# Softmax sums taken off the probabilities and put on the attention output, with kept weight slices and a one-instruction leaky step

## The reference

```
scores = q @ k.T / 8          # per head
keep   = (key < 4) or (0 <= row - key < 128)
a      = exp(scores - max);  a = a / (sum(a) + 1e-9)
x      = a @ v                # reshaped to 1536 tokens x 512
h = x @ w_in;   g = max(0.01 * h, h);   x = g @ w_out      # first layer, 512 -> 2048 -> 512
h = x @ w_in2;  g = h * sigmoid(h);     y = g @ w_out2     # second layer
```

## Time and profile before

| | us |
|---|---|
| median of 3 runs | 679.57 (679.01 to 680.44) |
| profiled execution, span from the first to the last instruction | 677.8 |
| PE busy | 634.3 |
| DVE busy | 415.4 |
| ACT busy | 362.4 |
| GpSimd busy | 99.3 |

### The profile page before, as it was taken

How to read it: one execution, slowest core, us unless ns; L and a number is a source line. 1 busy time by engine, 2 the same in 40 slices (tenths; PEclk the granted TensorE clock), 3 DMA queues, 4 the chain that set the end, 5 groups by cost and what they waited for, 6 DMA issues and landing times.

```text
span 677.8 us, 9233 instructions
## 1 busy us (share of the span) xinstructions
PE 634.3 (94%) x3048; PEld 529.2 (78%) x3048; DVE 415.4 (61%) x894; ACT 362.4 (53%) x788; POOL 99.3 (15%) x133
## 2 busy tenths in 40 slices
PE   2566799999999999999999999999999999999997
PEld 2565678888887778888888888888888888888886
DVE  7999977888888887886654545333343333433332
ACT  4667766666667666664544446443344434443342
POOL 5544422222324232200000000000000000000000
PEclk9977799999999999999999999999999999999999
DMA  6343981211121120000222221000010000100001
GB/s 145 110 113 111 297 261 34 47 48 33 48 47 33 48 63 17 1 1 1 93 94 93 94 94 31 1 0 1 1 62 1 0 1 1 58 6 0 1 1 62
DMA packets 12334, 36.50 MB, mean 54 GB/s; under 512 B 2048, under 2 KB 2048, under 8 KB 12288
## 3 DMA queue, kind: packets, MB, share of 16 engines
q1 hardware_dynamic: 12288, 35.92, 18.1%
HBM read 32.77 MB, written 3.15 MB: 53 GB/s over the span
## 4 chain that ended last, share of the span: by engine, by line
PE 62%; DVE 22%; ACT 8%; issue 6%; DMA 1%; ACTq 0%; SPq 0%; DVEq 0%
PE y_ps L808 29%; PE h_ps L781 29%; DVE sm L515 4%; DVE prob L597 4%; DVE pT L524 3%; DVE g_f L559 3%; ACT g L428 2%; ACT g_f L417 2%; DVE g L569 2%; DVE x L537 2%; DVE psT L529 1%; DVE row_inv L590 1%; PE o_ps L748 1%; ACT prob L355 1%; ACT win L400 1%
## 5 line engine op out<-in xcount | busy, mean ns | idle before, releaser
L781 PE MATMUL h_ps<-x,win 128*128 128x512 f32 x1152 | 284.0, 391 | 0.5 <-DVE win L544 0.5
L781 PEld LDWEIGHTS h_ps<-x,win 128*128 128x128 f32 x1152 | 212.8, 188 | 42.6 <-DVE win L544 0.8
L808 PE MATMUL y_ps<-g,wout 128*128 128x512 f32 x576 | 145.7, 393 | 0.0
L808 PE MATMUL y_ps<-wout,g 128*128 128x512 f32 x576 | 138.2, 389 | 0.0
L569 DVE TENSOR_TENSOR g<-g_f,g 128x512 fp32r<-128x512 f32 x96 | 70.9, 739 | 91.7 <-ACT g L421 85.4
L551 DVE TENSOR_TENSOR wout<-w_raw,wout 128x512 fp32r<-128x512 f32 x96 | 72.4, 754 | 86.9 <-ACT wout L408 86.7
L808 PEld LDWEIGHTS y_ps<-wout,g 128*128 128x128 f32 x576 | 108.1, 188 | 22.5
L808 PEld LDWEIGHTS y_ps<-g,wout 128*128 128x128 f32 x576 | 103.9, 188 | 18.6
L408 ACT ACTIVATE wout<-w_raw 128x512 fp32r<-128x512 f32 x96 | 60.2, 627 | 90.9 <-PE y_ps L808 90.9
L355 ACT ACTIVATE prob<-sm,neg_max 128x260 f32<-128x260 f32 x96 | 48.7, 508 | 43.3 <-DVE neg_max L515 42.7
L419 ACT ACTIVATE g_f<-h_ps 128x512 f32<-128x512 f32 x48 | 28.7, 598 | 69.3 <-PE h_ps L781 69.3
(11 more groups left out here) (72 smaller groups left out, 507.2 us busy)
## 6 DMA issues: line engine op xcount, KB each, us to landing
w_raw<-w SPq DMA_DIRECT2D x32, 512.0 KB, 3.5
qk_raw<-qk SPq DMA_DIRECT2D x48, 260.0 KB, 4.2
v_raw<-vt SPq DMA_DIRECT2D x12, 256.0 KB, 2.6
y<-qk_raw SPq DMA_DIRECT2D x12, 256.0 KB, 2.2
vs_raw<-vsink SPq DMA_DIRECT2D x8, 8.0 KB, 3.5
```

The costliest lines, as they stand in the source:

```text
L781: ins = mm(h_ps[:, :], win[:, F % 2, wp, c * P:(c + 1) * P], x[:, xp, c, i * BLK:(i + 1) * BLK], start=(c == 0 and wp == HI and xp == HI), ...
L808: ins = mm(y_ps[d][:, :], a[:, d * P:(d + 1) * P], r, start=(f == 0 and wp == HI and gp == HI), stop=(f == FT - 1 and wp == LO))
```

## The change

- The probabilities are no longer scaled. `exp` writes its sums of four heads side by side; for each half tile DVE adds 1e-9 and takes the reciprocal of the four columns, written 64 times each (128x256). PE turns that into two 128x128 blocks, in the same bank as the turned sinks; DVE copies them to SBUF (`scale`), and multiplies the output bank by them into `att` (`scale_half`). ACT rounds `att` into `x`, and GpSimd takes the low part. The high part of the turned sinks moves from ACT to DVE.
- The first tile of each batch element (tiles 0 and 6) has only its own 128 key columns: its scores, masks, exps, transposes and products leave out the rest. Tiles 0 and 1 of each element have no separate sink products.
- Weight slices are split into a store of eight slots. A block goes through the slices in the opposite order of the one before, so that the last eight of a block are still there: 64 splits instead of 96. The raw slices come through a ring of four buffers, one load per split.
- Leaky: ACT applies Prelu with slope 0.01 twice from the bank, as it does Silu in the second layer; `leaky` and `round_g` are gone.
- The first layer step is placed at tick 19 instead of 20, and the orders on all engines are written anew.

```diff
+        if F % FT < FT - KEPT or b == NB - 1:
+            del resident[layer, f]
+            free.append((split_slot[j], F))
...
+        if s < FT:
+            at, at_out = s - 4, s - 3
+        elif i < FT - KEPT:
+            at = at_out = s - 6
+        else:
+            i -= FT - KEPT
+            at = start + 2 + i + i // 2
+            at_out = at + 1
...
-            def normalise(u):
-                dve.wait_ge(exp_done, 2 * u + 2)
-                at = (2 * u) % PR
-                nc.vector.tensor_scalar_add(row_inv[:, u % 2, 0, :], row_sum[:, at:at + 2],
-                                            1e-9).then_inc(norm_step, 1)
-                dve.wait_ge(norm_step, 2 * u + 1)
-                nc.vector.reciprocal(row_inv[:, u % 2, 1, :], row_inv[:, u % 2, 0, :]).then_inc(norm_step, 1)
-                dve.wait_ge(norm_step, 2 * u + 2)
-                for i in range(2):
-                    a = prob[:, at + i, :]
-                    nc.vector.tensor_scalar(a, a, row_inv[:, u % 2, 1, i:i + 1], None,
-                                            ALU.mult).then_inc(prob_ready, 1)
...
+            def take_half(e):
+                k = job["half", e]
+                dve.wait_ge(t_written, k + 1)
                 bank_ = t_bank(k)
+                if has_sinks(e // 2):
+                    wait(dve, o_done, e)
+                    nc.vector.tensor_copy(psT[:, :], bank_[:, 2 * P:3 * P]).then_inc(sink_step, 1)
+                nc.vector.tensor_copy(scale[:, :, :], bank_[:, 0:2 * P].rearrange("p (c n) -> p c n", c=2)).then_inc(
+                    scale_ready, 1)
+                if has_sinks(e // 2):
+                    dve.wait_ge(sink_step, sunk(e) + 1)
+                    low = psT[P // 2:P, :]
+                    ins = nc.vector.tensor_tensor(low, bank_[P // 2:P, 2 * P:3 * P], low.bitcast(F32), ALU.subtract)
+                    ins.then_inc(t_ready, 1)
                 else:
+                    dve.wait_ge(scale_ready, e + 1)
+                    dve.sem_inc(t_ready, 1)
+            def invert_sums(e):
+                dve.wait_ge(exp_done, 4 * (e + 1))
+                wait(dve, t_written, job["half", e - 1] + 1 if e else 0)
+                nc.vector.tensor_scalar_add(sum_eps[:, :], row_sum[:, e % 2, :], 1e-9).then_inc(norm_step, 1)
+                dve.wait_ge(norm_step, 2 * e + 1)
+                nc.vector.reciprocal(row_inv[:, :, :],
+                                     sum_eps[:, :].unsqueeze(2).to_broadcast([P, H // 2, D])).then_inc(norm_step, 1)
+            def scale_half(e):
+                dve.wait_ge(o_done, e + 1)
+                dve.wait_ge(scale_ready, e + 1)
+                wait(dve, x_ready, e)
                 for lo in (0, D):
+                    src = o_bank(e)[lo:lo + D, :].rearrange("p (c n) -> p c n", c=2)[:, :, 2 * lo:2 * lo + P]
+                    ins = nc.vector.tensor_tensor(att[lo:lo + D, :, :], src, scale[lo:lo + D, :, :], ALU.mult)
+                ins.then_inc(att_ready, 1)
...
             def take_hidden(F):
+                func, slope = (ACT.Prelu, 0.01) if F < N_L0 else (ACT.Silu, 0.0)
                 act.wait_ge(h_done, F + 1)
                 wait(act, g_ready, F - 1)
+                nc.scalar.activation(g_f32[:, F % 2, :], h_ps[:, :], func, alpha=slope)
                 wait(act, y_done, F - 1)
+                nc.scalar.activation(g[:, 0, F % 2, :], h_ps[:, :], func, alpha=slope).then_inc(h_taken, 1)
...
+            def turn_half(e):
+                k = job["half", e]
+                wait(pe, t_ready, freed(t_bank, k))
+                pe.wait_ge(norm_step, 2 * e + 2)
+                bank_ = t_bank(k)
+                for c in range(2):
+                    src = row_inv[:, 2 * c:2 * c + 2, :].rearrange("p h d -> p (h d)")
+                    ins = nc.tensor.transpose(bank_[:, c * P:(c + 1) * P], src, ident[:, :])
+                if has_sinks(e // 2):
+                    pe.wait_ge(sinkp_ready, sink_at[2 * e + 1] + 1)
+                    src = prob_sink[:, e % 2, :, :, :].rearrange("p r h s -> p (r h s)")
+                    ins = nc.tensor.transpose(bank_[:, 2 * P:3 * P], src, ident[:, :])
+                ins.then_inc(t_written, 1)
...
+            for a in range(LAST):
+                head = a < FS
+                F = a - FS
+                if head:
+                    mask_max(2 * a)
+                    mask_max(2 * a + 1)
+                if a in inverted_in:
+                    invert_sums(inverted_in[a])
+                if 2 <= a <= NPAIR + 1:
+                    low_pair(a - 2)
+                if not head and a < NPAIR:
+                    mask_max(2 * a)
+                if a in turned_in:
+                    take_half(turned_in[a])
+                if a in scaled_in:
+                    scale_half(scaled_in[a])
+                if a == 4:
+                    stack_sink_values()
+                if a == FS:
+                    low_g(0)
+                if not head:
                     evacuate(F - 1, 1)
+                    if a < NPAIR:
+                        mask_max(2 * a + 1)
+                for s in wout_in.get(F, ()):
+                    low_wout(s)
+                if not head:
                     low_g(F + 1)
+                for s in win_in.get(F, ()):
+                    low_win(s)
+                if not head:
                     evacuate(F, 0)
...
+                if a < NPAIR:
+                    scores(2 * a)
+                if a == FS:
+                    hidden(0, 0)
+                    hidden(0, 1)
+                hidden(F + 1, 0)
+                if a in turned_in:
+                    turn_half(turned_in[a])
+                hidden(F + 1, 1)
+                if a < NPAIR:
+                    scores(2 * a + 1)
+                if a <= NPAIR + 1:
+                    weigh_values(a - 2)
+                project(F, 0)
+                if a <= NPAIR:
+                    turn_pair(a - 1)
+                if a in turned_in and has_sinks(turned_in[a] // 2):
+                    weigh_sinks(turned_in[a])
+                project(F, 1)
```

More of the change, by code:

```diff
@@ L54, in sink_window_attention_two_ffn @@
     SCALE = 1.0 / float(D) ** 0.5
-    LEAD = TB + 1
     REP = P // (H * NS)
-    assert D == 64 and HD == 512 and REP == 4 and window <= P and NS <= P and NF >= 2
-    job = {}
[L61 to L68, removed]
+    BLK = 512
+    TB = BLK // P
@@ new lines, in has_sinks @@
+    def has_sinks(T):
+        return T % TPB >= 2
+    NHALF = NPAIR // 2
+    sink_pairs = [u for u in range(NPAIR) if has_sinks(u // PAIRS)]
+    sink_at = {u: i for i, u in enumerate(sink_pairs)}
+    turned_in = {2 * e + 3: e for e in range(NHALF)}
+    inverted_in = {2 * e + 2: e for e in range(NHALF)}
+    scaled_in = {2 * e + 4: e for e in range(NHALF)}
+    job = {}
+    for a in range(LAST):
+        if a in turned_in:
+            job["half", turned_in[a]] = len(job)
+        if 1 <= a <= NPAIR:
+            job["pair", a - 1] = len(job)
@@ L130, in freed, with tokens @@
             return next((k + 1 for k in range(i - 1, -1, -1) if bank_of(k) is bank_of(i)), 0)
-        w_loaded = [sem(f"w_loaded{f}") for f in range(FT)]
+        def tokens(F):
+            b = steps[F][1]
+            return slice(b * BLK, (b + 1) * BLK)
+        w_loaded = [sem(f"w_loaded{r}") for r in range(RING)]
         qk_loaded = [sem(f"qk_loaded{i}") for i in range(2)]
@@ L225, in _ @@
                             sp.dma_start(vs_raw[r * n:(r + 1) * n, b, :], vsink[b]).then_inc(vs_loaded, 16)
[L226 to L253, removed]
+                if PAIRS <= a < 2 * PAIRS:
+                    load_w(a - PAIRS)
+                load_ws(a - FS)
+            for F in range(LAST - FS, NSTEP):
+                load_ws(F)
+                i, f = divmod(F - N_L0, FT)
+                if i > 0 and f == 1:
+                    store(i - 1)
+            store(NB - 1)
             for t in range(TB):
@@ L332, in _ @@
             low_v(0, 0)
-            for u in range(NPAIR + 1):
+            for u in range(LAST):
                 T, j = divmod(u, PAIRS)
@@ L375, in high_v, with high_pair @@
                 nc.scalar.activation(v_hl[:, T % TPB % 2, 0, part], v_raw[:, part], ACT.Copy).then_inc(v_high, 1)
-            def high(kind, i):
-                k = job[kind, i]
+            def high_pair(u):
+                k = job["pair", u]
                 act.wait_ge(t_written, k + 1)
[L380 to L386, removed]
@@ L744, in weigh_values @@
                 if u % 2 == 0:
-                    wait(pe, x_ready, freed(o_bank, e))
-                for s in range(2):
+                    wait(pe, att_ready, freed(o_bank, e))
+                only = not has_sinks(T)
+                slots = (0,) if width(T) == P else (0, 1)
+                for s in slots:
                     for vp, pp in PASSES:
```

584 lines of the change are left out of this document (261 added, 323 removed).

## The result

The changed kernel takes 689.84 us (median of 4 runs, 688.40 to 690.53) against 679.44 for the kernel before, measured beside it (4 runs, 679.01 to 680.44): a ratio of 1.0148, 95% interval 1.0136 to 1.0160. It is slower by 10.4 us, where the forecast was 665 and the range ended at 680. The span of the profiled execution is 688.3 against 677.8. A few executions of this and later comparisons ran far slower, at 811 us and more; medians leave them out.

A forecast was written before the change was run, and what follows sets the result against it. DVE was taken to bound the head, PE the rest: first layer product at 75.5, layers 522.2, attention 57.1, losses 5.0, stores 3.8, outside 1.8, together 665 us; range 654 to 680.

The forecast's parts named there:

- the losses behind it: PE's waits after the first layer product: 2 us at the handover and 0.2 per two ticks, 5.0 (3.5 to 11).
- the place of the reciprocal in DVE's even tick: DVE's reciprocal, low pT, mask, scaling: done at some 2.8 us, before PE wants the output bank at 3.4.
- the tick of the head as a sum of DVE's instructions: Head, before layer products: DVE's work gives 6.4 us per two ticks; first layer product at 75.5, 10.5 earlier.
- r: Time of DVE's 128x256 reciprocal of the sums: 1.4 us taken, ends 0.42 and 2.2.
- that rival: Output bank's return, decided by DVE's even-tick chain from r = 2.2 or equal loss beside GpSimd; 0.4 more: 688; chance 0.12.
- Beginning in tick 19 brings no gain of its own.: First layer step one tick earlier: a tick only goes from the head's 3.9 us to PE's 1.9.
- Kept slices "by itself worth nothing": Layer steps after 15 split half the weight slices; no gain, since ACT and DVE are not the bound there.
- the doubled weight transfers are hidden: Weights fetched 64 times instead of 32, hidden by three ticks or more of lead; uncovered, some 3 us a slice.
- Prelu needs no further table: ACT's leaky step; rival: two table loads of 1.28 us per tick, 671 to 740; chance 0.05 with the rest.
- PE's own budget: PE's attention work from the first layer product on: 57.1 us, beside 522.2 of layer products.
- The narrow tiles: Tile 6 at its own 128 key columns saves PE 2.6 us; tile 0's four head ticks take 2.6 each.
- nothing there is due within two ticks: SP's queue: sink loads move behind tile 1's first half, weight loads to ticks 4 to 7, without a near deadline.

The follow-up runs named there:

- the short one on DVE and ACT: Changed kernel with DVE's reciprocal of 128x4 and ACT copying it out to 128x256, first layer step at tick 19: 671.11 us; with tick 20, 668.21.
- The best version: Changed kernel with a 128x4 reciprocal on DVE, its copy to 128x256 on ACT, and the first layer step at tick 20: 668.21 us, ratio 0.9833.

## Why the prediction was wrong

By the forecast's own sum, the first product came at 81.6 instead of 75.5, which is 6.1 us, and the losses behind it were 684.44 - 81.61 - 522.2 - 57.1 = 23.5 us where 5.0 stood, which is 18.5. Together they are the 24.6 by which PE ended too late. The two steps that failed are the place of the reciprocal in DVE's even tick, and the tick of the head as a sum of DVE's instructions. The late reciprocal in the mixed ticks alone brings the losses from 23.5 to 12.9; with the short one on DVE and ACT and the start at tick 20 they are 5.4 (660.31 - 77.48 - 522.2, less 55.2 for one tick fewer).

**The place of the reciprocal: the step that failed.** I wrote "PE wants it 3.4 us into the even tick, DVE is done at some 2.8 for r up to 1.4", and put the point from which DVE's chain decides at r = 2.2. The reciprocal's duration was between my ends, and for this shape the rows read (count, ns min/median/max, start to end):

```profile
L563 DVE RECIPROCAL row_inv<-sum_eps x24: 1752/1753/1755, 13.2 to 318.2; 128x256 f32<-128x256 f32 x24
```

r = 1.75, not 1.4. The even tick of the changed kernel, at 129.64 on PE (timeline, all engines):

```profile
129.19 0.85 POOL L335 TENSOR_TENSOR v_hl<-v_raw,v_hl 128x256 fp32r<-128x256 f32 x1 [5.07 <-ACT v_hl L423]
129.36 0.71 DVE L561 TENSOR_SCALAR sum_eps<-row_sum 128x4 f32<-128x4 f32 x1
129.64 0.33 PE L695 MATMUL s_ps<-k_hl,q_st 128*128 128x128 f32 x2
130.10 1.75 DVE L563 RECIPROCAL row_inv<-sum_eps 128x256 f32<-128x256 f32 x1
131.78 0.63 DVE L535 TENSOR_TENSOR pT<-t_ps,pT 128x512 fp32r<-128x512 f32 x1
132.32 0.28 DVE L527 CUSTOM_DVE_ANT_0 sm<-s_ps,mask 128x128 f32<-128x128 f32 x1
132.52 0.85 DVE L572 TENSOR_TENSOR att<-o_ps,scale 64x256 f32<-64x256 f32 x2
132.64 0.40 ACT L404 ACTIVATE prob<-sm,neg_max 128x128 f32<-128x128 f32 x1 [3.53 <-DVE neg_max L527]
132.75 0.41 PE L695 MATMUL s_ps<-k_hl,q_st 128*128 128x128 f32 x2
133.52 0.71 PE L740 MATMUL o_ps<-pT,v_hl 128*128 128x256 f32 x4 [0.36 <-DVE att L572]
```

The scaling ends at 133.37, 3.7 us after the tick's first scores. That is my 2.8, if two terms are put right: 0.35 for r, and 0.55 because the addition takes 0.71 beside GpSimd instead of 0.16. PE wanted the bank at 133.16, 3.5 after the scores, close to my 3.4. So the place and both quantities were in the text, the addition's wait too ("with as much lost beside GpSimd"), but I set the threshold for the reciprocal alone and gave the case 0.12. The threshold was also miscounted: 2.8 at r = 1.4 reaches 3.4 at r = 2.0 and not 2.2, and at 2.2 the scaling would be 0.2 late and not 0.4. I also priced it by the bank alone. The listed wait for it is only 2.2 us; the same chain delays the low pT that the turning bank waits for (3.1 us), and the mask, for which ACT's exp waits 3.53 us here. With the chain freed, those waits go together, and 10.7 us with them. The 688 of that rival is near what happened, but its parts are not: r at 2.2 with 0.4 more puts the first product at 86.7 and the losses at 17, and they were 81.6 and 23.5. That the sum came close is luck.

The Trainium skill (VectorE: DVE Perf Modes, the pipeline's walkthrough) gives reciprocal a repeat count of 8, from which I estimated 2.1 us above the fixed part; the trace has 1.6 (1753 less 166 ns). The page's figure led to 0.5 us too much, my middle reading to 0.35 too little.

**The head.** Two ticks were 5.0 + r = 6.75 with the true r (my terms add up to 5.1); from mask to mask the rows have 46.09 to 53.11, 7.02. That sum was nearly right. Tick 8 begins at 35.80 and not 34.3, which is the first two tiles, and tick 15 at 60.13 and not 56.7: of the further 1.9, 1.2 are r. From there I had 18.8 us to the first product, four ticks with a slice of 4.5 and 0.8, and it took 21.5. DVE's first masks of these ticks and of tick 19 come at 60.13, 64.58, 71.29, 75.62 and 85.39: the odd ticks have about my 4.5, the even ones, with the reciprocal, have not (6.7 and 9.8). PE's clock was low here (0.51 from 70 to 75 us), but PE did not set the pace: it waited for DVE. Tick 16, of 6.7 us:

```profile
65.77 1.75 DVE L563 RECIPROCAL row_inv<-sum_eps 128x256 f32<-128x256 f32 x1
67.99 0.84 DVE L572 TENSOR_TENSOR att<-o_ps,scale 64x256 f32<-64x256 f32 x2
68.12 1.65 PE L740 MATMUL y_ps<-pT,v_hl 128*128 128x256 f32 x6 [3.80 <-DVE pT L535]
68.86 0.42 ACT L435 ACTIVATE x<-att 128x256 fp32r<-128x256 f32 x1 [2.71 <-DVE att L572]
69.19 0.61 ACT L447 ACTIVATE wout<-w_raw 128x512 fp32r<-128x512 f32 x1
69.83 0.81 DVE L584 TENSOR_TENSOR wout<-w_raw,wout 128x512 fp32r<-128x512 f32 x1 [1.00 <-ACT wout L447]
70.57 0.69 DVE L578 TENSOR_TENSOR win<-w_raw,win 128x512 fp32r<-128x512 f32 x1
71.29 0.43 DVE L527 CUSTOM_DVE_ANT_0 sm<-y_ps,mask 128x260 f32<-128x260 f32 x1
```

The work goes round a ring in which each engine takes its instructions in order: DVE scales, ACT rounds `x` and only then the slices, DVE subtracts the slices and only then begins the next mask. ACT idles 2.71 us in it, DVE 1.00, PE 3.80. I had added up DVE's instructions; in such a tick that is only a lower bound.

**"Beginning in tick 19 brings no gain of its own."** It brings a loss: 3.7 us with the long reciprocal, 2.9 with the short one. The block's first step then waits for a chain over DVE, ACT and GpSimd in its own tick (3.6 us in two blocks, and 1.5 more at the low clock behind the first), and the handover takes 15.1 us for what costs PE 10.1 (a step and a half, 8.2, and a tick's 1.9). Of the 5.0 between them 3.0 are a wait and some 1.6 the 3.2 us at half the clock behind it. There the wait is for ACT, which is held by an exp whose mask DVE reaches only at 85.39, behind two slices and a low pT (the slices' subtractions take 1.27 and 1.82 us beside GpSimd's, instead of 0.69):

```profile
85.39 0.42 DVE L527 CUSTOM_DVE_ANT_0 sm<-s_ps,mask 128x260 f32<-128x260 f32 x1
...
85.85 0.51 ACT L404 ACTIVATE prob<-sm,neg_max 128x260 f32<-128x260 f32 x1 [3.13 <-DVE neg_max L527]
...
86.36 0.58 ACT L454 ACTIVATE g_f<-h_ps 128x512 f32<-128x512 f32 x1
...
87.56 2.05 PE L774 MATMUL h_ps<-x,win 128*128 128x512 f32 x6 [3.00 <-ACT g L456]
```

**Kept slices "by itself worth nothing".** 3.2 us with the short reciprocal, 11.3 with the long one. I judged by the engines' busy shares, which are not what limits a tick. A slice costs when the in-order DVE reaches the next tick's chain late by it. The other half of that step, that the doubled weight transfers are hidden, holds: no list of waits has one for them.

**Right.** Prelu needs no further table, and leaky's leaving is a gain, 3.0 us alone. The last stretch keeps its 2.72 us per half step. PE's own budget stood as well: with the short reciprocal and tick 20 the mixed stretch has only 2.0 us of idle PE, and late in it two ticks take the 14.9 that I had named (267.67 to 282.56). The narrow tiles gave 1.6 us where I had 2.6 on PE alone.

**Open.** Medians do not separate the narrow tiles' 1.6 us well. The best version's median is still 3 us above the forecast of 665. Its rows show 2.2 us of ACT waiting for a load of q and k in the head, where I had written of SP's queue that "nothing there is due within two ticks"; no version tried to move that load. The exact share of each cause in the changed kernel's 18.5 us of losses is not shown either: in four mixed ticks PE idles for 1.5 us, but they take 2.4 longer than with the late reciprocal.

## What to carry to other kernels

In an order written out by hand, ask of each new instruction what stands behind it on its engine and who waits for that, and place the one with the latest reader last; the same 1.75 us, moved behind what was due, gave 12.8 us back. Its length still counts where that engine sets the pace: in the head 1.25 us less on DVE for each two ticks brought another 5.9. An engine that is 62% busy (136.6 of 219 us) can still set the time, so compare dates within a tick and not busy shares, and price work that is added to an idle engine by the tick it falls in. A stage may begin too early: where its first step reads the product of the same tick, one tick later was faster twice. In the changed kernel two waits of PE of some 3 us outside the head were each followed by some 3 us at half its clock, and so cost about half as much again.

## What was not expected of the hardware

- The reciprocal costs 6.25 ns for each further element: 166 ns for 128x2, 1753 for 128x256, which is (1753 - 166) / 254. The row of 128x4 has 178. Its spread is 3 ns over 24 instructions.
- It does not wait beside GpSimd, where neighbours of the same engine do. In one head tick of the changed kernel:

```profile
49.31 0.68 DVE L561 TENSOR_SCALAR sum_eps<-row_sum 128x4 f32<-128x4 f32 x1
50.02 1.75 DVE L563 RECIPROCAL row_inv<-sum_eps 128x256 f32<-128x256 f32 x1
50.03 1.30 POOL L326 TENSOR_TENSOR k_hl<-qk_raw,k_hl 128x528 fp32r<-128x528 f32 x1
```

- The copy of 128x256 from SBUF to SBUF does wait: 1.25 us beside a subtraction of 1.30 and 0.295 alone on DVE, 0.40 on ACT beside the same work. The engine with the longer copy was the faster place for it.
